# Attention, soft MoE and gated MLP on one core: both units of a tile attended at once, k turned behind probs

## The reference

```python
def _attn_ref(q, k, v):            # each (4, 8, 576, 64), float32
    scores = scale * np.matmul(q, k.transpose(0, 1, 3, 2))
    # bias = -slope[h] * |i - j|; only keys with 0 <= i - j < 128 count
    scores = np.where(mask, scores + bias[None], -1000000000.0)
    attn = np.exp(scores - max); attn = attn / (sum + 1e-09)
    return np.matmul(attn, v)
def _moe_ref(x, phi, w1, w2):      # x (2304, 512), 32 slots, 8 experts
    logits = x @ phi
    # softmax over tokens mixes x into 32 slots, each expert runs relu(s @ w1) @ w2 on 4 slots,
    # softmax over slots mixes them back
def _moe2_ref(x, w_in, w_out):     # d_ff 2048
    h = x @ w_in; return ((h * np.clip(h + 3.0, 0.0, 6.0) / 6.0) @ w_out)
```

## Time and profile before

| | |
|---|---|
| median of 3 runs | 457.27 us |
| the profiled execution | 456.89 us, span 455.2 us |
| TensorE matmul, busy | 419.4 us (92%) |
| TensorE weight load, busy | 341.4 us (75%) |
| VectorE, busy | 233.8 us (51%) |
| ScalarE, busy | 212.5 us (47%) |
| GpSimd, busy | 70.9 us (16%) |
| one exponential (L397) | 391 ns, 160 of them |

### The profile page before, as it was taken

How to read it: one execution, slowest core, us unless ns; L and a number is a source line. 1 busy time by engine, 2 the same in 40 slices (tenths; PEclk the granted TensorE clock), 3 DMA queues, 4 the chain that set the end, 5 groups by cost and what they waited for, 6 DMA issues and landing times.

```text
span 455.2 us, 10183 instructions
## 1 busy us (share of the span) xinstructions
PE 419.4 (92%) x3764; PEld 341.4 (75%) x3764; DVE 233.8 (51%) x698; ACT 212.5 (47%) x601; POOL 70.9 (16%) x112
## 2 busy tenths in 40 slices
PE   3899999999999968896596999999999999999997
PEld 2788888878888844575465788888888888888885
DVE  2467686777677745040434554445444445444442
ACT  2788777777777600000615434433343433343431
POOL 1133133223223302000575200000000000000000
PEclk9999999999999987999897999999999999999999
DMA  9759989799898373999900010101010101010101
GB/s 176 192 147 259 238 241 233 232 219 255 214 278 239 110 275 119 386 385 396 374 8 1 1 46 1 46 0 46 0 46 0 46 0 46 0 46 0 46 1 48
DMA packets 75494, 61.41 MB, mean 135 GB/s; under 512 B 57792, under 2 KB 57792, under 8 KB 75456
## 3 DMA queue, kind: packets, MB, share of 16 engines
q1 hardware_dynamic: 75456, 60.89, 44.3%
HBM read 56.16 MB, written 4.72 MB: 134 GB/s over the span
## 4 chain that ended last, share of the span: by engine, by line
PE 85%; DVE 6%; ACT 4%; issue 3%; DMA 1%; SPq 0%; DVEq 0%; ACTq 0%
PE probs_turned L957 23%; PE out_turned L957 22%; PE scores L756 7%; PE probs_turned L765 4%; PE out_turned L781 4%; PE scores L939 4%; PE scores L885 4%; PE scores L900 3%; PE routes L811 3%; PE out_turned L785 3%; PE turns L739 2%; PE turns L796 2%; ACT probs L397 2%; PE turns L731 2%; PE routes L835 1%
## 5 line engine op out<-in xcount | busy, mean ns | idle before, releaser
L683 DVE SCALAR_TENSOR_TENSOR g<-u,scores 128x512 f32<-128x512 f32 x72 | 49.5, 688 | 110.5 <-ACT u L435 110.5
L440 ACT ACTIVATE g_hi<-g 128x512 fp32r<-128x512 f32 x72 | 45.5, 633 | 120.4 <-PE out_turned L957 120.2
L957 PE MATMUL probs_turned<-w_out_hi,g_hi 128*128 128x512 f32 x144 | 58.0, 403 | 7.3 <-DVE g_lo L689 3.9
L397 ACT ACTIVATE probs<-probs,rowmin 128x128 f32<-128x128 f32 (+1 forms) x160 | 62.0, 391 | 3.5 <-DVE rowmin L508 3.5
L957 PE MATMUL probs_turned<-w_out_lo,g_hi 128*128 128x512 f32 x144 | 57.8, 402 | 0.0
L957 PE MATMUL probs_turned<-w_out_hi,g_lo 128*128 128x512 f32 x144 | 57.0, 396 | 0.0
L957 PE MATMUL out_turned<-w_out_hi,g_hi 128*128 128x512 f32 x144 | 56.8, 394 | 0.0
L957 PE MATMUL out_turned<-w_out_lo,g_hi 128*128 128x512 f32 x144 | 56.7, 394 | 0.0
L957 PE MATMUL out_turned<-w_out_hi,g_lo 128*128 128x512 f32 x144 | 56.7, 393 | 0.0
L689 DVE TENSOR_TENSOR g_lo<-g,g_hi 128x512 fp32r<-128x512 f32 x72 | 53.4, 741 | 3.1 <-ACT g_hi L440 3.1
L756 PE MATMUL scores<-k_t,q_t 64*128 64x128 f32 (+2 forms) x576 | 42.7, 286 | 0.8 <-ACT k_t L375 0.8
(11 more groups left out here) (131 smaller groups left out, 626.9 us busy)
## 6 DMA issues: line engine op xcount, KB each, us to landing
weight_ring<-in_moe_w_dram SPq DMA_DIRECT2D x32, 1024.0 KB, 7.7
out_dram<-y SPq DMA_DIRECT2D x18, 256.0 KB, 2.0
q_in<-in_q_dram SPq DMA_DIRECT2D x16, 256.0 KB, 4.4
k_in<-in_k_dram SPq DMA_DIRECT2D x16, 256.0 KB, 4.8
v_in<-in_v_dram SPq DMA_DIRECT2D x16, 256.0 KB, 3.9
weight_ring<-in_moe_w_in_dram SPq DMA_DIRECT2D x8, 512.0 KB, 12.5
weight_ring<-in_moe_w_out_dram SPq DMA_DIRECT2D x4, 1024.0 KB, 15.3
q_in<-in_q_dram SPq DMA_DIRECT2D x4, 128.0 KB, 4.1
```

The lines of the kernel that those rows point to most:

```text
L397: act.activation(probs[0:R, m % 2, h, :], probs[0:R, m % 2, h, :], ACT.Exp, bias=rowmin[0:R, m % 2, h:h + 1], scale=-1.0, accum_out=rsum[0 ...
L440: act.activation(g_hi[:, p % 2, :], g_sb[:, p % 4, :], ACT.Copy).then_inc(ghi_ready, 1)
L683: dve.scalar_tensor_tensor(out=g_sb[:, p % 4, :], in0=u_sb[:, p % 2, :], scalar=6.0, in1=bank[p % 4], op0=ALU.min, op1=ALU.mult).then_inc( ...
L957: ins = pe.matmul(bank[4 + kk][:, :], g[:, p % 2, cols], w[:, c, :], start=(p == 0 and i == 0 and a == 0), stop=(p == FPAIRS - 1 and i == ...
```

## The change

In even periods TensorE turns q, then probs, then k; before it was probs, q, attend, k. In odd periods it attends for both units of tile (m - 3) / 2 right behind the scores, ahead of turn_probs, turn_o and route; before each period had one attend, the last or last but one of its groups. ScalarE copies q, then probs, then k within the even period; before it was probs and q, and k at the head of the next one.

```diff
@@ scalar
             for m in range(LAST):
                 if m % 2 == 0 and 0 <= m // 2 - 2 < NT:
                     copy_out(m // 2 - 2)
-                if m % 2 == 1 and turns_in(m - 1) is not None:
-                    turn_k(turns_in(m - 1))
                 if batch_at(m, SOFT_AT) is not None:
                     soften(batch_at(m, SOFT_AT))
+                if turns_in(m) is not None:
+                    turn_q(turns_in(m))
                 if 1 <= m <= UNITS:
                     copy_probs(m - 1)
                 if turns_in(m) is not None:
-                    turn_q(turns_in(m))
+                    turn_k(turns_in(m))
                 if m < UNITS:
                     exps(m)
@@ tensor
             for m in range(LAST):
                 if m < UNITS:
                     scores(m)
+                if m % 2 == 1 and 0 <= m - 3 < UNITS:
+                    attend(m - 3)
+                    attend(m - 2)
+                if turns_in(m) is not None:
+                    turn_q(turns_in(m))
                 if 1 <= m <= UNITS:
                     turn_probs(m - 1)
                 if batch_at(m, SPREAD_AT) is not None:
                     spread_max(batch_at(m, SPREAD_AT))
                 if batch_at(m, SUM_AT) is not None:
                     sum_slots(batch_at(m, SUM_AT))
-                if turns_in(m) is not None:
-                    turn_q(turns_in(m))
                 if output_in(m) is not None:
                     turn_o(output_in(m))
                     route(output_in(m), m)
-                if 2 <= m <= UNITS + 1:
-                    attend(m - 2)
                 if batch_at(m, CMAX_AT) is not None:
                     turn_max(batch_at(m, CMAX_AT))
                 if turns_in(m) is not None:
```

## The result

The changed kernel takes 459.88 us, the median of 6 runs (459.26 to 462.14); the kernel before takes 457.28 (456.67 to 457.90). The ratio is 1.0068, 95% interval [1.0041, 1.0095]. Forecast was 456.1, within 453.8 to 459.4, so it went the other way, and 0.5 us beyond the range. The profiled execution is the slowest of the six, 462.14 us with a span of 460.4; a second profile of the same kernel (459.72 us, span 458.0) is near the median. I use both; they differ above all in when TensorE's clock falls.

A forecast was written before the change was run, and what follows sets the result against it. TensorE's issue was taken to bound the attention loop. Start -0.3, steady pairs -2.1, tail +0.6 and +0.7 for y in 17 odd periods gave -1.1 us, hence 456.1 us, range 453.8 to 459.4.

The forecast's parts named there:

- What bounds the loop, and the borders: Attention loop: TensorE sets the pace; a border between groups of different array shape costs about 0.2 us, behind route 0.07.
- x: Border from scores to attend: cost beyond the usual 0.2 us, bounded by 0 and 0.2, taken as 0.
- y: Border from route to scores: cost beyond 0.07 us, bounded by 0 and 0.13, taken as 0.04.
- rival B: Heads of first attend and of scores behind route: borders cost more, 459.4 us with x 0.1, y 0.13; chance 0.25.
- The even period: Even period without attend: q to k takes 1.33 us, with 0.55 of new wait; 3.00 after, 0.72 less.
- The odd period: Odd period with two attends, 0.82 and 1.02 us: 4.80 after against 3.98 before, 0.82 more.
- The pairs that aren't ordinary: The 16 steady pairs, including first-tile, 64-row, exponential-wait and slot-sum pairs: together -2.1 us.
- The start: First three tiles: exponentials decide more than TensorE, and the earlier scores give some back, -0.3 us.
- Rival C: Steady loop: ScalarE becomes the bound, each of 18 pairs gives 0.2 us of wait, 459.8 us; chance 0.07.
- The tail: Last scores to last turn of o: 10.2 us, 1.6 more, less 1.0 from period 38's lost attend: +0.6.
- It passes on in full: Behind the loop, up to the weights' ring and the end: the whole -1.1 us reaches the total time.
- A: The forecast itself: 456.1 us, from 454.9 to 457.4; chance 0.44, of which 0.6 falls on faster.

The follow-up runs named there:

- the two experiments on it: Changed kernel with exponentials ahead of k's copy in period 0 alone, 459.28 us; changed kernel with k's copy behind the exponentials in every period, 458.10 us.
- the filled kernel before: The kernel before plus extra matmuls of 128 columns, results unused, in TensorE's gaps behind the last attends: 454.66 us, ratio 0.9946.
- the early q: q turned at the end of the odd period, added to the changed kernel with start and last tile as before: 457.96 us, ratio 1.0021.
- the better order of the loop: Changed kernel with k's copy behind exponentials, last tile unpaired, q turned early: 451.52 us with extra matmuls, 457.72 us without them.

## Why the prediction was wrong, step by step

**What bounds the loop, and the borders: right.** TensorE's issue, and 0.2 us where two groups differ in array shape. x and y measured 0 and 0; I had 0 and 0.04, and rival B, at 0.25, falls. The Trainium skill (TensorEngine Tiling (Array Packing), Key Properties) says that a change of tiling mode drains TensorE. Priced like the other borders, that would have made route to scores 0.13 dearer; it is 1.04, so behind route the trace shows no such price, as in the earlier trace rows.

**The even period: right.** 1.34 from q to k. **The odd period: mis-sized by 0.05**, 1.89 for two attends and not 1.84; I had spread the first three groups' 0.61 evenly, but the first of a run takes 0.16 and each later one 0.22. The one ordinary pair among the 16 (periods 8 and 9) came out at +0.15 for +0.12. The waits of the earlier trace rows were not all of the loop's: 1.2 us for q's copy came on top.

**The pairs that aren't ordinary: two of five kinds mis-sized.** From the starts of the scores in both timelines, each kind of pair, us against before:

```
                                             forecast   measured
4 that turn a 64-row tile                    -0.46      -0.30
3 that attend a 64-row tile                  +0.52      +0.45
3 that attend a batch's first tile           -0.05      +0.27
3 that had a wait for exponentials           -0.35      -0.40
2 with the slot sums                         -0.38      -0.30
1 ordinary                                   +0.12      +0.15
sum of the 16                                -2.1       -0.7
```

So of the 1.4 that are missing 0.95 lie in the first-tile pairs and 0.6 in those that turn a 64-row tile; the others come to -0.2. For the 64-row tiles it isn't shown which term was off. In the first-tile pairs the turned probs wait, in all three:

```profile
57.28 0.97 PEld L756 LDWEIGHTS scores<-k_t,q_t 64*128 64x128 f32 x16 [0.17 <-issue]
58.37 0.85 PEld L785 LDWEIGHTS out_turned<-pt_diag,v_in 128*64 128x64 f32 x16
59.57 0.42 PEld L765 LDWEIGHTS probs_turned<-ident,probs 128*128 128x128 f32 x4 [0.34 <-ACT probs L397]
```

Two attends of half length are 0.85 us, too short for exponentials that now stand behind k's copy. I had reckoned ScalarE from the odd period's turn only ("from the start T of a turn of probs in an odd period"), never from k's turn in the even one. With k's copy back behind the exponentials each of these pairs is 0.18 shorter, so this is a good half of the 0.32 by which I missed them.

**The start: the step that failed most.** "The earlier scores give some of it back: -0.3"; it was +1.8. In ScalarE's queue k's copy moved ahead of exps(m), and at the start, where TensorE has nothing else to do, each wait of ScalarE for k is paid in full. I had costed the reordering of ScalarE at nothing ("I cost it at nothing, up to 0.1 a pair if I am off") and named slack of the steady state as its cover; the first periods have no such slack. By the two experiments on it k's copy costs 1.1 us in period 0, 0.2 in period 3 and 0.5 in the first-tile pairs, 1.8 in all. The rest of the start is the pairing itself in periods 4 and 5 (+0.37, k's copy back or not) and, in periods 2 and 3, the time at which TensorE reaches its later pace, which changes between executions. Rival C was near the total, 459.8, but put the price on 18 steady pairs.

**The tail: right at full clock, +0.7 against +0.6.** What was missing is the clock. "It passes on in full" took everything behind the last turn of o as fixed. In the second profile the steps up to the ring are 0.5 longer, with the clock falling some 2.6 us behind the last turn of o and not 4.8 as before (worked out from the shares of the 2 us stretches above); what follows is 0.5 longer too, for no cause shown. In the first profile there are another 0.65 up to the ring, and 1.8 inside the tail.

**The sum.** Start 2.1, pairs 1.4 less the 0.7 of borders that didn't come, tail 0.1, 1.0 behind the tail: 3.9 above the forecast -1.1, the +2.8 of the second profile. The medians differ by 2.6. The forecast's chances don't add up either: with the rest of A on same, its rivals give faster 0.41, same 0.31 and slower 0.28, not 0.46, 0.29 and 0.25.

What stays open: what decides in an execution whether the clock falls at 160 or at 166. In the same kernel both occur. Of the changed orders with extra matmuls, the two with a gap of 0.41 us between the last attends had a fall near 160 in their profile, and the two without it had none; but the filled kernel before had waits of 0.38 and 0.30 at its last turn of probs and attend, and no fall. So that filling the gaps keeps the clock up is shown, and which gap matters isn't. Nor did I try the early q in the unpaired order of the kernel before.

## What to carry to other kernels

Reckon a reordered queue three times: steady, from its first period, and through its last, because slack of the steady state covers nothing where the pipeline fills or drains. Of a copy that moves ahead of other work on its engine, ask what it waits for at its earliest, and who stands behind it meanwhile. Where the loop hands over to a short serial chain of small steps, look at the granted clock in each 2 us: small matmuls in its gaps, cut to the gaps, gave 2.6 us here by themselves, and the better order of the loop paid (3.1 us more) only together with them.

## What was not expected of the hardware

The clock fell to 1.2 GHz at 161 us in one execution and at 167 in another of the same kernel; ahead of the early fall no wait of TensorE in the tail was longer than 0.72 us. A float32 matmul of 128x128 weights takes some 0.89 us for 512 columns at full clock, and one of 128 columns 0.23 (eight in 1.86), so it fits a gap that the other overfills. At the start the same four loads of a turn of q took 0.71 us at 18.51 in one execution and 0.42 at 18.41 in another with the same queue up to there. That a border's price goes by the group in front held at every new border: 0.2 behind scores, attends and turns, 0.07 behind route.
